# Three edits to the attention stage of a fused attention and MLP kernel: first transfers in halves, decays and states on other engines, one product moved

## The reference

```python
# q, k, v: (2, 8, 768, 64)
for t in range(S):
    state = gamma[h] * state + outer(k[:, :, t], v[:, :, t])
    y[:, :, t] = scale * q[:, :, t] @ state
x = y.transpose(0, 2, 1, 3).reshape(1536, 512)
x = gelu_sigmoid(x @ moe_w_in) @ moe_w_out                  # 512 -> 2048 -> 512
xn = x / rms(x) * moe2_rms_g
x = (silu(xn @ w_gate) * (xn @ w_val)) @ w_out              # 512 -> 1536 -> 512
```

## Time and profile before

| | |
|---|---|
| median of 3 runs | 583.98 us (583.65 to 584.08) |
| profiled execution | 583.44 us, of which the span of instructions is 581.6 us |
| TensorE busy | 573.3 us (99%) |
| VectorE, ScalarE, GpSimd busy | 359.2, 298.1, 172.1 us |
| attention ends (first MLP matmul) | at 50.4 us |

### The profile page before, as it was taken

The page is one execution under the profiler, slowest core; times in us unless marked ns, Lnnn a source line. Parts: engine busy times, 40 slices in busy tenths (PEclk is TensorE's granted clock), DMA queues, the critical chain, the costliest instruction groups (busy, mean ns, idle before and its releaser), DMA issues.

```text
span 581.6 us, 9400 instructions
## 1 busy us (share of the span) xinstructions
PE 573.3 (99%) x3640; PEld 551.8 (95%) x3640; DVE 359.2 (62%) x486; ACT 298.1 (51%) x501; POOL 172.1 (30%) x222
## 2 busy tenths in 40 slices
PE   7999999999999999999999999999999999999997
PEld 7988999999999999999999999998889999998886
DVE  5797555676425667775346768678755666666432
ACT  1244766645336766645237655574444555564321
POOL 2386444000222452000314464410051545420000
PEclk9999999999999999999999999999999999999999
DMA  8981222322112222312202222233213322224202
GB/s 319 392 292 37 74 72 73 108 73 73 38 36 73 72 74 70 111 39 72 73 0 74 73 74 72 74 84 99 73 36 125 93 73 73 73 74 112 69 1 108
DMA packets 24220, 52.84 MB, mean 91 GB/s; under 512 B 1776, under 2 KB 1904, under 8 KB 24176
## 3 DMA queue, kind: packets, MB, share of 16 engines
q1 hardware_dynamic: 23600, 50.41, 28.2%
q10 hardware_dynamic: 576, 1.84, 0.8%
HBM read 49.09 MB, written 3.15 MB: 90 GB/s over the span
## 4 chain that ended last, share of the span: by engine, by line
PE 97%; DVE 1%; DMA 1%; issue 0%; ACT 0%
PE bank L539 20%; PE twin L539 20%; PE twin L480 11%; PE twin L483 11%; PE twin L482 11%; PE bank L483 6%; PE bank L480 6%; PE bank L482 6%; PE twin L392 2%; PE bank L438 2%; PE bank L425 1%; DMA arena<-attn_in 1%; PE bank L409 1%; DVE x_lo L787 0%; PE bank L580 0%
## 5 line engine op out<-in xcount | busy, mean ns | idle before, releaser
L778 DVE TENSOR_TENSOR w_lo<-raw,w_hi 128x512 fp32r<-128x512 f32 (+2 forms) x148 | 149.3, 1024 | 49.7 <-ACT w_hi L612 49.5
L1059 POOL TENSOR_TENSOR raw<-raw 128x256 f32<-128x256 f32 x40 | 32.1, 803 | 317.1 <-DMA raw<-w 312.5
L480 PE MATMUL twin<-x_hi,w_hi 128*128 128x384 f32 x360 | 120.5, 335 | 0.6 <-ACT arena L676 0.6
L483 PE MATMUL twin<-x_hi,w_lo 128*128 128x384 f32 x360 | 120.3, 334 | 0.0
L482 PE MATMUL twin<-x_lo,w_hi 128*128 128x384 f32 x360 | 120.2, 334 | 0.0
L612 ACT ACTIVATE w_hi<-raw 128x512 fp32r<-128x512 f32 (+2 forms) x148 | 109.0, 763 | 18.0 <-PE bank L539 7.6
L813 DVE TENSOR_TENSOR g_lo<-arena,g_hi 128x768 fp32r<-128x768 f32 x56 | 54.3, 970 | 74.8 <-ACT g_hi L642 74.8
L642 ACT ACTIVATE g_hi<-arena 128x768 fp32r<-128x768 f32 x56 | 47.5, 848 | 103.6 <-PE bank L539 103.6
L480 PEld LDWEIGHTS twin<-x_hi,w_hi 128*128 128x128 f32 x360 | 67.6, 188 | 0.9 <-ACT arena L676 0.9
L482 PEld LDWEIGHTS twin<-x_lo,w_hi 128*128 128x128 f32 x360 | 67.6, 188 | 0.0
L483 PEld LDWEIGHTS twin<-x_hi,w_lo 128*128 128x128 f32 x360 | 67.6, 188 | 0.0
(11 more groups left out here) (105 smaller groups left out, 995.9 us busy)
## 6 DMA issues: line engine op xcount, KB each, us to landing
raw<-w SPq DMA_DIRECT2D x68, 512.0 KB, 3.7
arena<-attn_in SPq DMA_DIRECT2D x22, 512.0 KB, 7.9
out<-x SPq DMA_DIRECT2D x1, 1536.0 KB, 8.6
out<-x SPq DMA_DIRECT2D x6, 256.0 KB, 2.0
arena<-attn_in ACTq DMA_DIRECT2D x2, 512.0 KB, 10.1
arena<-tables ACTq DMA_DIRECT2D x1, 512.0 KB, 6.1
arena<-tables ACTq DMA_DIRECT2D x1, 256.0 KB, 9.8
ident<-ident_in SPq DMA_DIRECT2D x1, 64.0 KB, 12.8
```

The source lines that it names most:

```text
L480: pe.matmul(dst, w_hi[q][:, w], x_hi[:, x], start=start and kk == 0, stop=False, skip_group_check=True)
L483: mm = pe.matmul(dst, w_lo[q][:, w], x_hi[:, x], start=False, stop=kk == 1, skip_group_check=True)
L778: dve.tensor_tensor(w_lo[q % 3][:, dst], src, w_hi[q % 3][:, dst].bitcast(F32), ALU.subtract)\
L1059: pool.tensor_tensor(s1, a21, a22, ALU.add).then_inc(w_sums, 1)
```

## The change

Five parts, and the names they have in the rows of the changed kernel:

1. The first transfers (q and k of steps 0 and 1, the mask, k and v of step 0) are each split into two, one on SyncE's queue and one on ScalarE's. Semaphores count 32 instead of 16 there.
2. Three fill matmuls become two ahead of `scores(1)` and four behind it. In the first pair `from_chunk(0)` now stands ahead of `new_products(0)`.
3. `decay_q` is VectorE's for all steps. Both are made in one place, after `masked(a + 1)`.
4. `new_state` is ScalarE's: one activation for a batch's first chunk, otherwise four, one for each pair of heads, since the scale of an activation is one number per partition.
5. The preparation for the MLP is placed anew: `sum_x(0, T1)` on VectorE now follows the two `decay_q` of its pair, `split_x(0, T1)` moves from the pair of step 8 to that of step 6, and `split_x(0, T2)` from that of 10 to that of 8. In the first unit M6 comes ahead of M3.

```diff
-FILL = 3
+FILL = (2, 4)
-LOWER = {True: (B11, B21, T1, B22, T3, T2, T4), ...
+LOWER = {True: (B11, B21, T1, B22, T2, T3, T4), ...
@@ SyncE
-            load(0)
-            load(1)
+            for a in range(2):
+                sp.dma_start(slot[a][:, 0:512], attn_in[BATCH * a, :, 0:512]).then_inc(qk_in[a], 16)
+            sp.dma_start(mask[:, 0:512], tables[:, T_MASK:T_MASK + 512]).then_inc(mask_in, 16)
+            sp.dma_start(slot[0][:, 1536:2048], attn_in[0, :, 1536:2048]).then_inc(kv_in[0], 16)
@@ TensorE
                 scores(a)
                 if a == 0:
-                    for _ in range(FILL):
-                        pe.matmul(gate[1][:, 0:P], ones[:, :], ones[:, :], start=True, stop=True)
+                    fill(FILL[0])
                 scores(a + 1)
                 if a == 0:
-                    new_products(0)
+                    fill(FILL[1])
                     from_state(0)
                     from_chunk(0)
+                    new_products(0)
@@ hidden(0, 0)
+                    product(6, n, 2, 1, 2, T2, False)
                     pe.wait_ge(m5_copied, n + 1)
                     product(3, n, 1, 1, 3, B22, False)
-                    product(6, n, 2, 1, 2, T2, False)
@@ ScalarE
+            for a in range(2):
+                act.dma_start(slot[a][:, 512:1024], attn_in[BATCH * a, :, 512:1024]).then_inc(qk_in[a], 16)
+            act.dma_start(mask[:, 512:1024], tables[:, T_MASK + 512:T_Q]).then_inc(mask_in, 16)
+            act.dma_start(slot[0][:, 1024:1536], attn_in[0, :, 1024:1536]).then_inc(kv_in[0], 16)
+            def new_state(a):
+                ...
+                if c == 0:
+                    ins = act.activation(state[m % 2], val[g][:, 0:256], ACT.Copy)
+                else:
+                    for p in range(PAIRS):
+                        at_ = PAIRS * c + p
+                        ins = act.activation(state[m % 2][:, cols(p, 64)], val[g][:, cols(p, 64)], ACT.Copy,
+                                             scale=state_decay[:, at_:at_ + 1])
+                ins.then_inc(state_done, 1)
                 elif a == 6:
                     split_x(0, B22)
                     split_w(0, 1)
+                    split_x(0, T1)
                 elif a == 8:
-                    split_x(0, T1)
                     split_x(0, T3)
                     split_w(0, 2)
-                elif a == 10:
                     split_x(0, T2)
-                copy_y(a)
+                if a == 0:
+                    copy_y(0)
+                    new_state(0)
+                new_state(a + 1)
+                if a > 0:
+                    copy_y(a)
                 copy_y(a + 1)
+                if a + 2 < STEPS:
+                    new_state(a + 2)
@@ VectorE
             for a in range(0, STEPS, 2):
                 masked(a)
+                masked(a + 1)
                 if a == 0:
                     decay_q(1)
-                    new_state(0)
-                masked(a + 1)
...
+                for b in (a + 2, a + 3):
+                    if b < STEPS and b % CHUNKS > 0:
+                        decay_q(b)
...
                 elif a == 6:
                     sum_x(0, T1)
+                    lower_x(0, T1)
                 elif a == 8:
                     lower_x(0, B22)
+                    sum_x(0, T2)
                     lower_w(0, 1)
```

More of the change, by code:

```diff
@@ L52 @@
 UPPER = {True: (B11, B21, B22, T1, T3, T2, T4), False: (B11, B21, T1, T2, B22, T3, T4)}
-LOWER = {True: (B11, B21, T1, B22, T3, T2, T4), False: (B11, B21, T1, T2, B22, T3, T4)}
+LOWER = {True: (B11, B21, T1, B22, T2, T3, T4), False: (B11, B21, T1, T2, B22, T3, T4)}
 SET = ((0, 1, 2), (3, 4, 5))
@@ L136, in transformer_kernel @@
         probs_done = sem("probs_done")
-        q_decayed = [sem(f"q_decayed{i}") for i in range(BATCH)]
+        q_decayed = sem("q_decayed")
         k_decayed = sem("k_decayed")
@@ L319, in set_decay, with qk_at, kv_at @@
             return ins
+        def qk_at(a):
+            return 16 * (a // SLOTS) + (32 if a % SLOTS < 2 else 16)
+        def kv_at(a):
+            return 16 * (a // SLOTS) + (32 if a % SLOTS == 0 else 16)
         block = ctx.enter_context(nc.Block())
@@ L360, in _ @@
                     sp.wait_ge(y_done, b - SLOTS + 1)
+                    if b == SLOTS:
+                        sp.wait_ge(kv_done, 1)
                     load_kv(b)
@@ L444, in _, with fill @@
             pe.wait_ge(ones_set, 1)
-            for _ in range(WARM_UP):
-                pe.matmul(gate[1][:, 0:P], ones[:, :], ones[:, :], start=True, stop=True)
+            def fill(count):
+                for _ in range(count):
+                    pe.matmul(gate[1][:, 0:P], ones[:, :], ones[:, :], start=True, stop=True)
+            fill(WARM_UP)
             for a in range(0, STEPS, 2):
@@ L701, in copy_y @@
                                ACT.Copy).then_inc(y_copied, 1)
+            def new_state(a):
+                g, c = chunk_of(a)
+                if c == CHUNKS - 1:
+                    return
+                m = state_at(a)
+                act.wait_ge(kv_done, m + 1)
+                if m >= 2:
+                    act.wait_ge(cross_done, m - 1)
+                if c == 0:
[6 more added lines that the diff above has]
+                ins.then_inc(state_done, 1)
+            act.wait_ge(factors_set, 2)
             for a in range(0, STEPS, 2):
@@ L897, in masked @@
                    .then_inc(probs_done, 1)
[L899 to L912, removed]
             def decay_q(a):
@@ L918, in decay_q @@
                     dve.wait_ge(q_table_in, 16)
-                dve.wait_ge(qk_in[r], 16 * (a // SLOTS) + 16)
+                dve.wait_ge(qk_in[r], qk_at(a))
                 if x >= 2:
                     dve.wait_ge(cross_done, x - 1)
-                dve.tensor_tensor(q_dec[x % 2], slot[r][:, 0:512], q_table, ALU.mult).then_inc(q_decayed[0], 1)
+                dve.tensor_tensor(q_dec[x % 2], slot[r][:, 0:512], q_table, ALU.mult).then_inc(q_decayed, 1)
             for a in range(0, STEPS, 2):
                 masked(a)
+                masked(a + 1)
                 if a == 0:
                     decay_q(1)
-                    new_state(0)
-                masked(a + 1)
-                if a < 4:
-                    decay_q(a + 2)
-                elif a == 4:
-                    lower_x(0, B11)
[L934 to L939, removed]
+                for b in (a + 2, a + 3):
+                    if b < STEPS and b % CHUNKS > 0:
+                        decay_q(b)
+                if a == 4:
+                    lower_x(0, B11)
                     lower_x(0, B21)
@@ L943, in _ @@
                     sum_x(0, T1)
+                    lower_x(0, T1)
                 elif a == 8:
                     lower_x(0, B22)
+                    sum_x(0, T2)
                     lower_w(0, 1)
[L947 to L950, removed]
+                elif a == 10:
+                    lower_x(0, T2)
+                    lower_x(0, T3)
                     lower_w(0, 2)
-                    lower_x(0, T3)
-                    lower_x(0, T2)
             for p, (layer, _) in enumerate(PHASES):
@@ L1073, in _ @@
             for a in range(0, STEPS, 2):
-                for b in (a, a + 1):
-                    if b > CHUNKS:
-                        decay_q(b)
                 if (a + 1) % CHUNKS < CHUNKS - 1:
```

27 lines of the change are left out of this document (7 added, 20 removed).

## The result

The changed kernel took **593.65 us** (median of 4 runs, 590.78 to 594.64) beside 583.82 us for the kernel before (4 runs, 583.5 to 584.08): ratio 1.0156, 95% interval 1.0138 to 1.0174. It is slower, as forecast; but by 9.8 us and not by 4.2, and above the range of 585.9 to 590.8.

The account below looks back on a forecast made before the run. TensorE was taken as the bound, nearly gapless from the MLP on, so attention's delay counts whole. +5.0 us at new_products(10) and -0.74 in the first MLP unit gave +4.2 on 583.98: 588.2 us, range 585.9 to 590.8.

Parts of the forecast that it names:

- What bounds the kernel: From the first MLP units on, TensorE is busy 520.6 of 523.8 us; attention's final delay is handed on whole.
- The new wait: ScalarE's splits of T1 and T2 await VectorE's sums, delaying states: new_products(8) +3.6 us, new_products(10) +5.0 us.
- first chain: From scores(6) at 31.05 through VectorE's sums and ScalarE's split of T1 to new_products(8) at 39.75, +3.6 us.
- masked(6) starts 1.20 after the scores: On VectorE, masked(6) begins 1.20 us after scores(6) begins at 31.05, so at 32.25.
- VectorE's neighbour: GpSimd's decay_k(8) and (9) add 0 to 2.1 us to VectorE's chain; overlap saves some 0.4 per chain; taken to cancel.
- rival 2: TensorE's clock falls to 1.2 GHz after both standstills, pairs of scores at half speed: +4.0 us, 592.2; chance 0.09.
- The start: Halved first transfers, six fills and the first pair's new order: +0.5 us at scores(6), bounds 0 and +1.5.
- rival 5: Halved transfers win nothing: scores(0) stays at 6.73, six fills shift all by another 1.5 us: 589.7; no separate chance.
- States on ScalarE: Four 128x64 activations for a state take 0.9 us, 0.23 each; bounds 0.42 and 1.96.
- The first unit: First MLP unit: M3 between M6 and M7 covers the copy, gap 0.91 becomes 0.17: -0.74 us.
- One chain hides: T1's sums ready in time, only the wait before new_products(10) stalls TensorE: 585.1, chance 0.06; both nearly hidden: 583.5, 0.05.
- Faster: Neither wait ahead of new_products(8) and new_products(10) is felt: -2.0 us, 582.0; chance 0.04.

Follow-up runs that it names:

- the first: Changed kernel with eight constant matmuls ahead of new_products(8) and four ahead of new_products(10) on TensorE: 590.78 us.
- the fitted fills: Changed kernel with 18 constant matmuls ahead of new_products(8) and 7 ahead of new_products(10) on TensorE: 590.07 us.
- the second experiment: Changed kernel with only the split of T1 moved behind the states, that of T2 left ahead of new_state(9): 590.56 us.
- the experiment on VectorE's order: Changed kernel with the sum for T1 ahead of decay_q(8) and decay_q(9) instead of behind them: 591.22 us.
- the longer: Changed kernel with 28 constant matmuls ahead of new_products(8) and 14 ahead of new_products(10) on TensorE: 593.41 us.
- the first experiment: Changed kernel with the splits of T1 and T2 both moved behind the states on ScalarE: 584.94 us.

## Why the prediction was right in kind and wrong in size

**What bounds the kernel.** Right: from 65 us on nothing differs, and attention's delay came through whole.

**The new wait.** Right, and shown: the two gaps are ahead of the instructions named, with the releaser named, and go when the two splits move (8.7 us). The step's own numbers were too small, in the profiled execution, the quickest of the four:

| first chain | predicted | measured |
|---|---|---|
| scores(6) start | 31.05 | 31.57 |
| masked(6) starts | 32.25 | 33.26 |
| two masked, two decay_q | 3.7 | 3.6 |
| two sums | 1.9 | 2.67 |
| split of T1, four activations | 1.75 | 1.66 |
| new_products(8) | 39.75 | 41.32 |

Two steps failed in this chain. One is the line "masked(6) starts 1.20 after the scores". I had read the 1.20 us at scores(4), where VectorE stood idle and waited for them. Ahead of masked(6) its list holds `lower_x` twice and `lower_w`, and the trace of the kernel before already had masked(6) 2.11 us behind scores(6) (30.54):

```profile
32.65 2.34 DVE L896 TENSOR_TENSOR arena<-twin,arena 128x1024 f32<-128x1024 f32 x2
```

In the changed kernel it was 1.69 us, and in the traces of the first and the fitted fills, whose chain is the same, 2.58 and 2.59. The other is the term called "VectorE's neighbour", where I let GpSimd's blocks (0 to 2.1 us) and the overlap cancel. They don't: the first sum took 1.79 us instead of 0.95, and the two `lower_x` and the `lower_w` ahead of masked(6) ran beside GpSimd's decay_k(6) and (7) and took longer than by themselves (1.80 us for the `lower_w`, 0.94 in the trace of the fitted fills). The Trainium skill ("SBUF — State Buffer", section on who interferes with whom) says that a VectorE operation with two SBUF inputs and a GpSimd operation that reads SBUF contend for a pair of ports which one of them holds alone, and that the order of issue decides who waits. The trace agrees: decay_k(9) ran from 36.69 to 37.80, and the sum that was issued at 36.82 ended 0.81 us after it. I had both numbers before me, and set a term with one sign to zero.

The range went wrong with it. Its high end took GpSimd's blocks for one chain only and left out the start's own upper bound of +1.5.

**The clock.** The step that failed most was rival 2, "The clock falls too", to which I gave 0.09. In the sum the clock was a term of nothing; it measured 3.0 to 3.8 us of the median (the fitted fills), near the +4.0 of that rival. The rival has the clock fall after both standstills. In the profiled execution it fell to 0.50 after the first (4.31 us) and not after the second; that it fell after both in slower runs is likely from their lower mean clock (0.991 instead of 0.994 in two of them), but it is not shown, as no trace is of such a run. My argument against it was that the clock had stayed at 1.00 through a standstill of 1.89 us; but I had just forecast standstills of 2.4 and 3.6 us, which no row of before covers, and a reading outside the rows is no evidence for the low chance. Nor was the 1.00 itself: the scores right behind the 1.89 us took 2.08 us for one step, which is half rate, as two steps take 2.06 us later. The page that I cited there, "TensorE: Matmul & The Clock Gate" of the Trainium skill, section on why this matters, pointed the other way with its warning of idle gaps, and the runs bear it out only in part (below). The two errors also feed each other: a longer standstill is likelier to lose the clock, and scores at half rate (3.35 us) make the next masked, and so the second chain, later by over 1 us.

**The start.** Predicted +0.5, measured +1.1. Its mechanism was wrong in part. I had priced fills and scores by rows between 6.7 and 12.4 us, 0.52 us a fill and 2.08 for one step's scores. Those ran at half rate, which I could have seen from the same group: two steps' scores take 2.06 us later on. In the changed kernel a fill took 0.29 and a step's scores 1.16. So TensorE was through its early work at 8.8 us, and stood 1.87 for k and v of step 0, which landed a microsecond later than before (decay_k(0) starts on them at 10.77 us instead of 9.68), with more halves ahead of them; then the clock was at 0.71 from 10 to 12 us and at 0.50 from 12 to 14. That halves win nothing (rival 5) was not so for the first operand, 1.9 us earlier; it was so for the stage.

**States on ScalarE.** Right: 0.91 us for four, 0.9 predicted from the line through the earlier trace rows. The 1.4 us worked out from the Trainium skill ("ScalarE: Activation LUTs", section on rules for kernel authors) is not what these runs show.

**The first unit.** Right, as far as the runs can tell: -0.64 in the trace of the changed kernel, -0.59 in that of the unit order alone, -0.5 by that kernel's runs (0 to -1.0); -0.74 predicted.

**The other rivals.** One chain hides (585.1) did not happen. The second experiment shows what it would have been: not 585, but 588 to 592, since the second chain alone stalls TensorE for 3.48 us. Faster (582.0) was out of reach; even without both waits and the start, the best is 583.4.

What stays open: why the clock falls in some runs of one kernel and not in others (588.06 us at 1.00 and 592.48 at 0.991 in the second experiment), and why k and v of some steps land more than a microsecond apart from run to run (decay_k(8), which waits for them, started at 34.71 us in the changed kernel and at 36.41 with the first fills), which moves VectorE's blocks. new_products(8) came 9.75 us after scores(6) in the changed kernel's trace, and 10.56 and 11.03 in those of the fitted and the first fills; so single traces compare these chains only to a microsecond. A first chain longer than in the profiled execution may also be a part of the 2.9 us between it and the median; no run separates that from the clock.

## What to carry to other kernels

Before an operation moves to another engine, look at what that engine stands still for just ahead of it: a wait that nobody felt becomes a wait of everything that is put behind it, and here two lines in another place were worth 8.7 us. The time from a result to the operation that uses it is read at the same place of the list, with what stands ahead of it there, and not at another step. When a forecast contains a standstill of TensorE longer than any in the profile, price the clock with it and give that case a real chance; constant matmuls fitted into the gap test it cheaply. And a known disturbance with one sign is added at its middle, never set against an unrelated saving.

## What the runs showed of the hardware that was not expected

- The granted clock reads 1.00 from the start in the kernel before, while scores(0) and the fills ran at half the rate seen elsewhere (2.08 us for a step's scores against 1.03 later on, 0.52 for a fill against 0.29 in the changed kernel). There the matmuls' own length is what to go by.
- The fall of the clock is not certain. After 4.31 us idle it was at 0.50, after 2.89 us too, and in another profiled execution 3.48 us idle passed at 1.00. Shorter gaps did not protect it: it fell behind the 2.02 us of the experiment on VectorE's order and behind the 1.87 us in the start of the changed kernel, while 2.02 us in the changed kernel's second chain and 1.88 us in the start of the first fills' trace passed at 1.00. It may be a part of the spread of a kernel's runs (3.9 us for the changed kernel, 0.5 and 1.7 with the longer and the fitted fills), but not the whole: the first experiment has no such gap, and its runs spread over 2.9 us.
- Four 128x64 activations in a row take 0.91 to 0.93 us, 0.23 each.
- A constant 128x128 float32 matmul, repeated, takes 0.23 to 0.26 us at full clock.
- The new order of the first transfers, in halves over two queues, brought the first operand some 1.9 us forward, and what lay behind it back: the mask's first use from 6.96 to 8.41 us, as VectorE's first row after it shows:

```profile
8.41 0.22 DVE L928 TENSOR_TENSOR arena<-arena 128x40 f32<-128x40 f32 x1 [3.16 <-DMA arena<-tables]
```
